# Two GpSimd drain instructions taken out of the expert stage of an attention and mixture-of-experts kernel

## The reference, cut to what matters

```python
# 1 linear attention with decay: B=4, H=8, S=768, D=48
for t in range(S):
    y[:, :, t] = r_t @ (state + (u * k_t) outer v_t)
    state = w * state + k_t outer v_t
x = y as rows                                  # [3072, 384]
# 2 dense layer: w_in [384, 2048], w_out [2048, 384]
h = x @ w_in
x = (h * sigmoid(h)) @ w_out                   # [3072, 384]
# 3 eight experts, one for each token: w1 [8, 384, 1024], w2 [8, 1024, 384]
logits = x @ w_gate + modality_bias[modality_id]
e_idx = argmax(logits); gate_w = softmax(logits)[e_idx]
for e in range(8):
    mask = e_idx == e
    out[mask] = gate_w[mask] * (relu(x[mask] @ w1[e]) @ w2[e])
```

## Time and profile before

| | us |
|---|---|
| median of 3 runs (lowest, highest) | 780.0 (779.23, 780.97) |
| the profiled execution, its own time | 780.97 |
| its span, first to last instruction | 779.4 |
| granted TensorE clock, mean of the span | 0.995 |
| PE busy | 744.3 |
| DVE busy | 502.1 |
| ACT busy | 421.5 |
| POOL busy | 235.3 |

### The profile page before, as it was taken

How to read it: one execution, slowest core, us unless ns; L and a number is a source line. 1 busy time by engine, 2 the same in 40 slices (tenths; PEclk the granted TensorE clock), 3 DMA queues, 4 the chain that set the end, 5 groups by cost and what they waited for, 6 DMA issues and landing times.

```text
span 779.4 us, 24925 instructions
## 1 busy us (share of the span) xinstructions
PE 744.3 (95%) x9894; PEld 724.9 (93%) x9894; DVE 502.1 (64%) x1348; ACT 421.5 (54%) x1076; POOL 235.3 (30%) x349
## 2 busy tenths in 40 slices
PE   3699999999999999999999999999998999999997
PEld 3598899999999999999999999999998899999997
DVE  7889665866676556766585657425774666666565
ACT  4776545545364555454555445445554556655564
POOL 4531222232224221332233201320223443334431
PEclk9999999999999999999999999999999999999999
DMA  8951221223222222232222210413465666656663
GB/s 313 389 186 40 93 80 59 82 71 98 76 97 76 97 63 76 74 97 77 96 77 64 85 63 23 164 61 121 184 164 202 232 225 245 227 202 212 239 236 121
DMA packets 24161, 104.95 MB, mean 135 GB/s; under 512 B 4412, under 2 KB 9801, under 8 KB 20483
## 3 DMA queue, kind: packets, MB, share of 16 engines
q1 hardware_dynamic: 19362, 93.34, 34.2%
q0 software_dynamic: 4704, 10.29, 3.9%
HBM read 93.90 MB, written 10.11 MB: 133 GB/s over the span
## 4 chain that ended last, share of the span: by engine, by line
PE 76%; DVE 9%; DMA 5%; issue 5%; ACT 3%; POOL 1%; POOLq 1%; SPq 0%; ACTq 0%; DVEq 0%
PE ps_h L1473 8%; PE ps_h L1474 8%; PE ps_h L1475 8%; PE ps_o L1490 7%; PE ps_o L1491 7%; PE ps_o L1492 7%; PE ps_s L1417 5%; PE ps_o L620 4%; PE ps_o L622 4%; PE ps_o L621 4%; DVE x_lo L1249 2%; DVE state L1264 2%; PE ps_y L593 2%; PE ps_y L595 2%; PE ps_y L594 2%
## 5 line engine op out<-in xcount | busy, mean ns | idle before, releaser
L1074 ACT ACTIVATE g<-ps_h 128x256 f32<-128x256 f32 x192 | 73.5, 383 | 205.3 <-PE ps_h L1475 175.3
L1473 PE MATMUL ps_h<-x_hi,wi_hi 128*128 128x256 f32 x576 | 165.5, 287 | 5.2 <-DVE x_lo L1249 5.2
L1474 PE MATMUL ps_h<-x_lo,wi_hi 128*128 128x256 f32 x576 | 163.0, 283 | 0.0
L1475 PE MATMUL ps_h<-x_hi,wi_lo 128*128 128x256 f32 x576 | 162.7, 282 | 0.0
L1490 PE MATMUL ps_o<-wo_hi,g_hi 128*128 128x392 f32 x384 | 136.0, 354 | 2.7 <-DVE g_lo L1282 1.5
L1491 PE MATMUL ps_o<-wo_lo,g_hi 128*128 128x392 f32 x384 | 131.4, 342 | 0.0
L1492 PE MATMUL ps_o<-wo_hi,g_lo 128*128 128x392 f32 x384 | 131.3, 342 | 0.0
L944 POOL TENSOR_TENSOR store<-store,up_half 128x256 f32<-128x256 f32 x44 | 34.1, 776 | 314.6 <-PE ps_y L1460 312.4
L1282 DVE TENSOR_TENSOR g_lo<-g,g_hi 128x256 fp32r<-128x256 f32 x192 | 82.4, 432 | 65.9 <-ACT g_hi L1067 64.0
L1473 PEld LDWEIGHTS ps_h<-x_hi,wi_hi 128*128 128x128 f32 x576 | 110.5, 192 | 7.2 <-DVE x_lo L1249 5.3
L1475 PEld LDWEIGHTS ps_h<-x_hi,wi_lo 128*128 128x128 f32 x576 | 110.9, 193 | 0.0
(11 more groups left out here) (205 smaller groups left out, 1607.2 us busy)
## 6 DMA issues: line engine op xcount, KB each, us to landing
store<-in_w SPq DMA_DIRECT2D x28, 1536.0 KB, 6.1
store<-in_quads SPq DMA_DIRECT2D x48, 704.0 KB, 4.4
x_rows<-rows SPq DMA_DIRECT2D x12, 384.0 KB, 3.2
woT_raw<-in_woT SPq DMA_DIRECT2D x4, 768.0 KB, 10.1
wi_raw<-in_wi SPq DMA_DIRECT2D x4, 768.0 KB, 10.4
wo_raw<-in_wo SPq DMA_DIRECT2D x4, 768.0 KB, 11.8
store<-x_rows,entries POOLq DMA_INDIRECT x26
out_rows<-y,entries_out POOLq DMA_INDIRECT x26
```

The source lines that it names most:

```text
L1074: S.activation(g[:, F % 2, :], ps_h[F % 2][:, 0:ETOK], ACT.Silu).then_inc(g_made, 1)
L1473: T.matmul(out, hi, x_hi[:, t % 2, c, :], start=(c == 0), stop=False)
L1474: T.matmul(out, hi, x_lo[:, t % 2, c, :], start=False, stop=False)
L1475: last = T.matmul(out, lo, x_hi[:, t % 2, c, :], start=False, stop=(c == KC - 1))
```

## The change

Two lines go. Nothing is put in their place, and the order of all other instructions stays.

```diff
@@ -399,7 +399,6 @@
         gather(0, z.x_rows[0:z.N - TOK, :])
         shift_entries(0)
         take_entries(1)
-        G.drain()
         for i in range(2):
             pool.wait_ge(z.rows_out[i], 16 * (z.N // ETOK // 2))
         gather(1, z.x_rows)
```

## The result

The changed kernel takes 784.86 us (median of 7 runs, 782.56 to 786.21) where the kernel before takes 780.38 (7 runs, 778.02 to 782.01): a ratio of 1.0055, interval 1.0035 to 1.0075. It is 4.5 us slower. The prediction had 778.3, and its range ended at 780.4.

A forecast was written before the change was run, and what follows sets the result against it. PE, busy 95% of the span, bounds the kernel; only one drain of twelve is on the path. Its 1.71 us stall gone, all else 0: 779.3 from the profiled 780.97, 778.3 from the median 780.0; range 777.3 to 780.4.

The forecast's parts named there:

- Removing it is worth 0: Drain ahead of the loop: removal gains 0, since POOL's next gather had waited 37.14 us for PE.
- So each is worth 0: Ten loop drains after the first: removal gains 0 each, as gathers wait for PE, have slack, or POOL waits for ACT.
- There are 12: Count of POOL's drains: one ahead of the loop, 2275 ns, and 11 in it; some 8 us in sum.
- no other instruction is a drain on POOL: Ground for excluding that the change doesn't do what it says: POOL has no drains but those removed.
- d = 1.23 us: After the loop's first pass: POOL's next instructions come 1.23 us earlier if the whole drain is dead time; lower bound 0.49.
- The gather gets ahead of the load: Second gather, issued at 604.31, is ready before the `w2` load's first packets and lands near 608, well before 611.00.
- The rival of the plain shift: Second gather keeps its 7.08 us to landing wherever it starts; gain 1.23 us, 778.8; chance 0.17.
- The full stall of 1.71 us: PE's stalled turn at 612.66 starts at 611.00 instead; all 1.71 us gained, 778.3; chance 0.52.
- The long drain's excess passes on to the next instruction: Rival: first loop drain's extra 0.74 us stays, d is 0.49; gain taken as 0.2 us, 779.8; chance 0.22.
- The gather last: Rival: second gather served last behind the weight load, landing at 613.66; PE turns 1.04 us later, 781.0; chance 0.09.
- something that the trace doesn't show: Unnamed cause, given 0.04 of the 0.07 chance of being slower by over 0.2%.
- Later turns follow each other as before: Sign of being right: PE's turns behind the stalled one keep their spacing.

The follow-up runs named there:

- e2: Kernel before with the loop's 11 drains taken out and the drain of line 402 kept: 779.51 us, ratio 1.0031 to the kernel before.
- e3: Changed kernel plus one drain behind the loop, ahead of the last results: 776.68 us, ratio 1.0002 to the kernel before.
- e1: Kernel before with only the drain of line 402 taken out, the loop's kept: 777.56 us, ratio 1.0000 to the kernel before.
- e6: Changed kernel plus a drain in each pass ahead of the wait for landed results: 776.81 us, ratio 0.9996 to the kernel before.
- e5: Changed kernel plus 16 DMAs on POOL, each reading 256 list entries into all 128 partitions: 784.49 us, run once.

## Why the prediction was wrong

Its mechanism at the stalled turn was right, and the sum was wrong because one term was missing. By its own steps:

- **"Removing it is worth 0" (line 402), "So each is worth 0" (the other ten): wrong, the step that failed.** The prediction took a drain for dead time that goes when the instruction goes. It has work to do, and that work stays: with the drain out, its 27, 14 or 5 DMAs are left to the next drain. Under POOL's long waits for PE and ACT this work had cost nothing; at the program's end nothing covers it. e2 shows line 402's part and e3 the place of the rest. The missing term is 8.71 - 2.28 = 6.43 us by the two drains' rows, 6.40 by the tail.
- **"There are 12" and "no other instruction is a drain on POOL": wrong.** There were 14, with one of 188 ns at the program's start and the one at the block's end, which the list of drains by line holds under a line that the diff does not touch. The clue stood in the earlier trace rows: three drains with nothing to tell them apart in the text, 2275, 1198 and 458 ns long. The prediction noted that "a drain's length depends on something else" and used it as a point for a rival about one drain, but never asked what it depended on. Counting the DMAs ahead of each would have given 0.08 us for one, 7.7 us for the last, and some 785.7 for the whole (780.97 - 1.71 + 6.4), against 785.89 profiled. That this comes so near is luck in part: in this pair of profiles the way from the first turn to the last gave 0.34 us and not 1.71, and the earlier start of 1.17 us, which is scatter, made up for most of it.
- **d = 1.23 us: right, a little small.** From the start of line 378's copy to the second gather's issue it was 1.46 us less. The idle time between that copy and line 363's is 0.90 us, and it was 2.13 by the same view before: 1.23 less. The other 0.23 are the copy of line 363 itself, 0.42 us before and 0.19 after.
- **The gather gets ahead of the load: right.** The packets by queue of the kernel after, for 602 to 604.5, 604.5 to 605.5, 605.5 to 606.5, and 606.5 to 609 us (packets, MB, share):

```profile
q0 software_dynamic: 88, 0.20, 28.7%
...
q0 software_dynamic: 41, 0.14, 52.3%
...
q1 hardware_dynamic: 18, 0.22, 93.9%
q0 software_dynamic: 31, 0.06, 15.8%
...
q1 hardware_dynamic: 71, 0.87, 102.5%
```

  The last packets of q0 lie ahead of 606.5, and then the load has the engines for itself. In the earlier trace rows q0 stood still likewise for 2.5 us, but with the gather behind it. e1 shows the other side: a gather whose first half is issued 1.35 us behind the load (602.61 - 601.26) doesn't get in between. What holds the gather back is not shown: the load's packets may go first, or the gather's own may be ready late while the load runs. The rival of the plain shift (1.23 us) was not what came, and the order of issue did matter. The Trainium skill's rule of turns, packet by packet ("DMA: Bandwidth & Descriptors", "Queues, rings and completion order"), need not speak against this, as the prediction had it: what the page calls a packet is a group of descriptors, 9 to 17 as a rule, and by the size of the profile's packets (78 for 0.96 MB) the load has, by an estimate, eight of them for each of 16 engines, which could be a single turn. No run shows whether it is.
- **The full stall of 1.71 us: right.** Turn to turn 1.76 us less. In this profile 1.4 of it are lost again in the neighbouring steps (17.24 to 17.55 and 18.89 to 19.04 ahead of it, 17.30 to 17.55 and 17.56 to 18.27 behind it). In the change's second trace the last of these is 17.55 again, and over all twelve steps that trace is 1.1 to 1.6 us shorter than those of the kernel before. So the stage gives about 1 us, with a scatter as large.
- **The rivals.** The gather keeps its 7.08 us: no. The long drain's excess passes on to the next instruction: no, though it was nearest to the truth, since the work does pass on, but to the next drain and not to the next instruction. The gather last: no. Slower it was, by a mechanism that was not among them, and the 0.04 for "something that the trace doesn't show" was for a thing that it did show.
- **The signs to look for** were met at the stalled turn: no drain, one wait for rows, the second gather's packets ahead of the load, a turn without a wait. "Later turns follow each other as before" was not met in this profile (17.56 to 18.27 above). All signs were placed within the stretch of the gain, and none at the program's end.

## What to carry to other kernels

Before an instruction that waits or flushes is taken out, ask what work it does and who does that work afterwards; different lengths of the same instruction are the question to start with. On POOL keep a drain where the engine waits anyway, and often enough that few DMAs are left for the last one: the best version here does 27 under a wait of 37 us, 64 under one of 9, and two at the end. And look at the program's last microseconds in both profiles, since there nothing covers anything.

## What the runs showed of the hardware

- A drain on POOL takes 0.055 us and 0.082 us for each DMA that POOL issued since its last drain, gather, scatter or plain load of 8 bytes alike. With 0.0819 that is a fit over five counts (5, 14, 27, 41 and 64), and within 12 ns of their rows. Four others (66, 91, 93 and 109) lie within 12 ns of it too, for the drains of the block's end less the 1.03 us in which the last issue still runs. It holds where the landing of the last of them doesn't take longer.
- It ends no sooner than the DMAs have landed (e6: 3.8 us for five, ending 0.2 to 0.3 us behind the landing), and it does its work while they are under way.
- It does not hold with 16 wide DMAs more: the last drain was 8.14 us where the count gives 10.0, and one late issue began 0.6 us late (e5). The cause stays open.
- A pass of the loop whose condition is false costs POOL some 0.5 us (six in 3.0 us, e3).
